# Another order of the weight loads and of the mix stage in a fused attention, soft-MoE and squared-ReLU kernel

## Chip, cores and metric

One Trainium2 chip, one of its cores. The metric is the device time of one launch in microseconds. A profiled execution also has a span, from the first to the last instruction of the trace. TensorE is called PE here, VectorE DVE, ScalarE ACT, GpSimd POOL, and SyncE, which issues most DMAs, SP.

## The reference

Three layers, each on the output of the one before, all in float32, for 4 x 576 = 2304 tokens of 512 features:

```python
# attention, 8 heads of 64, causal window of 128, ALiBi bias
scores = where(mask, q @ k.T / 8 + bias, -1e9)
x = softmax(scores) @ v                      # -> x [2304, 512]
# soft MoE, 8 experts of 4 slots, F = 1024
logits = x @ phi                             # [2304, 32]
slot_input = softmax(logits, axis=0).T @ x   # [32, 512]
slot_out[e] = relu(slot_input[e] @ w1[e]) @ w2[e]
x = softmax(logits, axis=1) @ slot_out       # [2304, 512]
# feed-forward, F = 2048
return relu(x @ w_in) ** 2 @ w_out
```

## The kernel before

All engines run their own program inside one block, and semaphores tie them together.

**Attention** takes 16 steps (4 batches x 4 pairs of heads). SP's loop (lines 401 to 409) issues in step n the v of step n, the k of step n+3, one half of a weight item, and the q of step n+4, all on one queue. PE works on scores, transposes of the probabilities and outputs (lines 938 to 1002; the q transposes are line 921), and the outputs land transposed in `xT`.

**Expert weights** are 16 items of 2 MB: item 2e is w1 of expert e, item 2e+1 its w2. They live in a ring of 8 slots (`RING`, line 31): six in `ring` (`EARLY`), two in `ring_late` at the top of SBUF. `load_half` (line 382) brings items 0 to 5 in twelve halves during attention steps 0 to 11; the first half of item 8, w1 of expert 4, goes to a tile `spare` after the loop (line 410). When the last attention output is done, `load_item` (line 338) brings items 6 and 7. Then come the four loads of w_in (lines 414 to 416, each after four more of the transposed tiles of x, since `win_sb` lies over `xT`), and then the other items in the order of `LATE_ITEMS` (line 34), each when the expert that used its slot is done (`e1_done`, `e2_done`), and last w_out in four loads (line 421).

**Slot inputs.** After attention PE forms the logits (line 1034), transposes x into rows (line 1045), adds up the slot inputs (line 1075), and turns them (line 1106).

**Expert loop** (lines 1162 to 1170). In round e PE does `expert_in(e)` (line 1127, w1), `expert_turn(e-1)` (line 1135), `expert_out(e-2)` (line 1148, w2), and, for the first five, `comb_turn(e-2)` (line 1158), which transposes the softmaxed mixing weights; DVE takes those into `combT` in `take_combT`. After the last expert DVE copies the slot outputs, PE turns them (line 1174) and DVE writes `soT`.

**Mix stage.** The product of slot outputs and w_in, 32 x 2048, is called mix and takes the place of w_in for all tokens. It is formed in four pieces of 512 columns. `mix_parts(n)` (line 1188) makes four partial products, ACT or DVE copies them (`take_part`), `mix_sum(n)` (line 1194) adds them, ACT rounds the sum into `mix` (line 864) and DVE writes the rest for its lower rows (line 708). `MIX_BANKS` names the two PSUM banks of each piece; before, the sum of one piece uses the bank of another's parts. `win_sb` holds w_in with row 4p+c on partition p, so the turn reads the slot outputs with a stride of four, which the copies of lines 632 and 693 put in order.

**Feed-forward.** Blocks of 256 tokens (`FT`), nine in all; a block has eight units u of 256 hidden features. `hidden` (line 1202) is the product of mix and combT for one unit; ACT does relu (line 876) and the rounded square (line 879), DVE the square (line 720) and its lower part (line 724); `project` (lines 1218 to 1220) is three products with the higher and lower parts of w_out, 12 instructions a unit. PE keeps `AHEAD` = 4 units of hidden ahead of the projections. w_out's parts are made in block 0: ACT rounds a unit of `wout_raw` to `wout_hi` (`split_high`, line 854), DVE subtracts (`split_low`, line 689). The order of these on each engine is written out by hand in `first` and `step`. POOL normalizes probabilities in attention (line 467) and clears `hidT`; after that it has nothing to do.

Of the kernel before, what the change touches and what calls it, by code (L numbers as in the profile page):

```python
# [5 lines left out]
F32 = mybir.dt.float32  # L6
F32R = mybir.dt.float32r
ALU = mybir.AluOpType
# [22 lines left out]
RING, RW = 8, 4096  # L31
EARLY = 6
ITEMS = 2 * E
LATE_ITEMS = (8, 10, 12, 9, 14, 11, 13, 15)
SPLIT_ITEM = 8
# [29 lines left out]
def attention_moe_ffn(nc, q, k, v, phi, w1, w2, w_in, w_out, out):  # L65
# [5 lines left out]
    win_v = w_in.rearrange("(p c) f -> c p f", c=DC)  # L71
# [4 lines left out]
    with ctx:  # L76
# [38 lines left out]
        wout_raw = sb("wout_raw", [P, FC, DM])  # L115
        place["at"] = ring_at
# [4 lines left out]
        assert place["at"] == ring_end  # L121

        spare = sb("spare", [P, RW // 2])

# [3 lines left out]
        xT_end = place["at"]  # L128
        place["at"] = xT_at
# [29 lines left out]
        ring_late = sb("ring_late", [P, RING - EARLY, RW])  # L159
# [7 lines left out]
        assert place["at"] <= late_at  # L167
# [9 lines left out]
        place["at"] = comb_end  # L177
        combT = sb("combT", [P, NTOK], F32R)
        assert place["at"] <= late_at
        place["at"] = late_at  # L180
        mix = sb("mix", [P, F2], F32R)
# [24 lines left out]
        spare_loaded = sem("spare_loaded")  # L206
# [74 lines left out]
        wsplit = sem("wsplit")  # L281
        l1_done = sem("l1_done")
# [52 lines left out]
        def ring_slot(slot):  # L335
            return ring[:, slot, :] if slot < EARLY else ring_late[:, slot - EARLY, :]

        def load_item(eng, i):
            e, slot = i // 2, i % RING
            if i >= RING:  # L340
                was = i - RING
                eng.wait_ge(e2_done if was % 2 else e1_done, was // 2 + 1)
            to = ring_slot(slot)
            if i % 2 == 0:
                cols = slice(RW // 2 if i == SPLIT_ITEM else 0, RW)
                eng.dma_start(to[:, cols], w1_v[e][:, cols]).then_inc(ring_loaded[slot], 16)
# [10 lines left out]
        def _(sp):  # L357
# [62 lines left out]
            for i in range(4):  # L420
# [15 lines left out]
        def _(pool):  # L436
# [43 lines left out]
            nc.gpsimd.memset(hidT[:, :, :, :], 0.0).then_inc(hidT_clear, 1)  # L480


        @block.vector
        def _(dve):
# [195 lines left out]
            for e in range(2, E):  # L680
                take_hidT(e)
                if e - 2 < QT:
                    take_combT(e - 2)

            def split_low(u):
# [7 lines left out]
            nc.vector.tensor_copy(slots_sb[:, :].rearrange("r (c x) -> r c x", c=DC),  # L693
                                  psum[:, BK_E2, :].rearrange("r (x c) -> r c x", c=DC)).then_inc(so_ready, 1)
# [16 lines left out]
            take_part(1)  # L711
            split_low(0)
            take_mix(0)
            take_mix(1)


# [12 lines left out]
            def first():  # L729
                low_part(0, 0)  # L730
                take_part(3)
                take_mix(2)
                low_part(1, 1)
                split_low(1)
                low_part(2, 2)
                take_mix(3)
                split_low(2)
                low_part(3, 3)
                split_low(3)

            def step(n, par):
                for u in range(AHEAD, FU):
                    if isinstance(n, int) and n == 0:
                        split_low(u)
                    low_part(FU * n + u, u)
# [11 lines left out]
        def _(act):  # L757
# [108 lines left out]
            take_part(0)  # L866
            split_high(0)
            take_mix(0)
            split_high(1)
            take_part(2)  # L870
            take_mix(1)

# [10 lines left out]
            def first():  # L883
                high_part(0, 0)
                high_part(1, 1)
                take_mix(2)
                split_high(2)
                high_part(2, 2)
                take_mix(3)
                high_part(3, 3)  # L890
                split_high(3)
                split_high(4)

            def step(n, par):
                for u in range(AHEAD, FU):
                    if isinstance(n, int) and n == 0 and u + 1 < FU:
                        split_high(u + 1)
                    high_part(FU * n + u, u)
# [11 lines left out]
        def _(pe):  # L910
# [204 lines left out]
            def expert_in(e):  # L1115
                i = 2 * e
                wait_item(i)
                if e >= 2:
                    pe.wait_ge(hid_ready, e - 1)
                w = ring_slot(i % RING).rearrange("p (c f) -> p c f", c=DC)  # L1120
                early_w = spare[:, :].rearrange("p (c f) -> p c f", c=DC // 2)
                if i == SPLIT_ITEM:
                    pe.wait_ge(spare_loaded, 16)
                for c in range(DC):
                    for j in range(4):
                        w_c = (early_w if i == SPLIT_ITEM and c < DC // 2 else w)[:, c, 2 * P * j:2 * P * j + 2 * P]
                        last = mm(psum[NS * j:NS * j + NS, BK_E1 + e % 2, 0:2 * P], siT[:, c, :], w_c, start=(c == 0), stop=(c == DC - 1))  # L1127
                last.then_inc(e1_done, 1)
# [32 lines left out]

            for e in range(E + 2):
# [4 lines left out]
                if e >= 2:  # L1167
                    expert_out(e - 2)
                    if e - 2 < QT:
                        comb_turn(e - 2)  # L1170

            pe.wait_ge(so_ready, 1)
            for c in range(DC):
                last = mm(psum[:, 1, NS * c:NS * c + NS],
                          slots_sb[:, P * c:P * c + P], fold[:, 0:NS],
                          start=True, stop=True)
            last.then_inc(soT_done, 1)
            pe.wait_ge(soT_ready, 1)


            for c in range(DC):
                pe.wait_ge(win_loaded[c], 16)

            def mix_parts(n):
                if n == 3:
                    pe.wait_ge(mix_ready, 1)
# [19 lines left out]
            def project(n, m, u, par):  # L1206
                pe.wait_ge(lo_done, m + 1)
                if isinstance(n, int) and n == 0:
                    pe.wait_ge(wsplit, u + 1)
# [13 lines left out]
            def first():  # L1223
# [6 lines left out]
                for u in range(AHEAD):  # L1230
                    if u % 2 == 0:
                        pe.wait_ge(mix_ready, u // 2 + 1)
                    hidden(0, u, u)
                    if u == 1:
                        mix_parts(3)
                        mix_sum(2)
                mix_sum(3)

            def step(n, par):
                for u in range(FU):  # L1240
                    if u < FU - AHEAD:
                        if isinstance(n, int) and n == 0:
                            pe.wait_ge(mix_ready, (u + AHEAD) // 2 + 1)
# [11 lines left out]
MIX_BANKS = ((4, 7), (5, 4), (6, 5), (7, 6))  # L1255
# [21 lines left out]
```

## Time and profile before

| | us |
|---|---|
| median of 3 runs | 442.83 (438.8 to 444.55) |
| profiled execution, its own time | 443.9 |
| its span | 441.9 |
| PE busy | 407.4 (92%) |
| DVE busy | 240.2 (54%) |
| ACT busy | 218.9 (50%) |
| POOL busy | 71.6 (16%) |
| mean granted PE clock | 0.98 |

Times in rows are microseconds from the start of the span. "x16" is a count of instructions merged into a row. PE is TensorE's matmuls, PEld its weight loads, SPq the queue of SP. The number in brackets behind a row is the idle time just before it and what ended it. In a row of windows each engine's busy time is followed by its count, then come the granted clock (1.00 is full), the mean busy share of the 16 DMA engines, and GB/s.

### The profile page before, as it was taken

The page shows a single profiled execution, that of the slowest core. Times are in us where ns is not written, and L with a number is a line of the kernel's source. Part 1 is how long each engine was busy: PE and PEld are TensorE (multiplying, and loading weights), DVE is VectorE, ACT ScalarE, POOL GpSimd, SP SyncE. Part 2 cuts the span into 40 slices and gives each one's busy share as a digit, 9 for nine tenths or more (in the row PEclk, how much of TensorE's full clock was granted, in tenths as well). Part 3 has the DMA queues.
Part 4 walks back from the last instruction along what each step waited for, and adds up shares of the span by engine and source line. Part 5 has one row for each costly group of instructions (what it writes and reads, how often), then busy time and mean ns, then how long its engine had stood idle before and what let it go on. Part 6 is the DMA issues. An engine that isn't in the chain of part 4 may idle for free.

```text
span 441.9 us, 7857 instructions
## 1 busy us (share of the span) xinstructions
PE 407.4 (92%) x2851; PEld 307.0 (69%) x2851; DVE 240.2 (54%) x680; ACT 218.9 (50%) x558; POOL 71.6 (16%) x61
## 2 busy tenths in 40 slices
PE   4799999799898988966999999999999999999996
PEld 3578787577676643421278888888888888888884
DVE  3888888687654544200499645454445445455530
ACT  2989889788753320100596434444434434444420
POOL 2374655554450010000000000000000000000000
PEclk9999999999999999986799999999999999999999
DMA  8799999899445969999400101010010101010101
GB/s 163 202 258 248 247 260 239 202 243 258 99 123 188 403 225 406 398 384 386 181 1 2 47 1 47 1 47 0 2 48 1 47 0 47 0 47 0 49 0 47
DMA packets 73411, 61.35 MB, mean 139 GB/s; under 512 B 58785, under 2 KB 58785, under 8 KB 71329
## 3 DMA queue, kind: packets, MB, share of 16 engines
q1 hardware_dynamic: 71264, 60.37, 44.9%
q10 hardware_dynamic: 2112, 0.52, 0.7%
q8 instruction: 21, 0.34, 0.3%
q14 instruction: 14, 0.11, 0.1%
HBM read 56.16 MB, written 4.72 MB: 138 GB/s over the span
## 4 chain that ended last, share of the span: by engine, by line
PE 74%; DMA 11%; SPq 5%; ACT 4%; DVE 3%; POOL 1%; issue 1%; DVEq 0%; ACTq 0%; POOLq 0%
PE psum L1219 15%; PE psum L1220 15%; PE psum L1218 15%; DMA q_in<-in_q 6%; DMA ring_late<-in_moe_w 4%; PE psum L1202 4%; PE psum L951 3%; PE psum L993 3%; PE psum L975 3%; ACT probs L764 3%; PE psum L1127 3%; PE psum L1045 2%; PE psum L1148 2%; PE psum L921 2%; PE psum L1075 1%; PE psum L1188 1%
## 5 line engine op out<-in xcount | busy, mean ns | idle before, releaser
L1220 PE MATMUL psum<-wout_hi,act_lo 128*128 128x512 f32 x288 | 113.3, 394 | 0.0
L1219 PE MATMUL psum<-wout_lo,act_hi 128*128 128x512 f32 x288 | 113.2, 393 | 0.0
L1218 PE MATMUL psum<-wout_hi,act_hi 128*128 128x512 f32 x288 | 112.4, 390 | 0.0
L720 DVE TENSOR_TENSOR sq_h<-relu_h 128x512 f32<-128x512 f32 x72 | 49.7, 691 | 81.5 <-ACT relu_h L876 81.3
L876 ACT ACTIVATE relu_h<-psum 128x512 f32<-128x512 f32 x72 | 43.1, 599 | 91.8 <-PE psum L1202 89.1
L467 POOL TENSOR_TENSOR probs<-probs,row_inv 128x1024 f32<-128x1024 f32 x31 | 59.2, 1929 | 56.2 <-DVE row_inv L558 56.2
L764 ACT ACTIVATE probs<-probs,row_min 128x256 f32<-128x256 f32 (+1 forms) x128 | 60.1, 471 | 13.8 <-DVE row_min L508 13.8
L1220 PEld LDWEIGHTS psum<-wout_hi,act_lo 128*128 128x128 f32 x288 | 54.0, 188 | 11.8
L1219 PEld LDWEIGHTS psum<-wout_lo,act_hi 128*128 128x128 f32 x288 | 54.0, 188 | 10.0
L1218 PEld LDWEIGHTS psum<-wout_hi,act_hi 128*128 128x128 f32 x288 | 54.1, 188 | 9.8
L724 DVE TENSOR_TENSOR act_lo<-sq_h,act_hi 128x512 fp32r<-128x512 f32 x72 | 49.9, 693 | 5.0
L879 ACT ACTIVATE act_hi<-relu_h 128x512 fp32r<-128x512 f32 x72 | 45.6, 633 | 4.3
L508 DVE CUSTOM_DVE_ANT_0 probs<-psum,rel 128x256 f32<-128x256 f32 (+1 forms) x128 | 42.1, 385 | 3.4 <-PE psum L951 3.4
L975 PE MATMUL psum<-ident,probs 128*128 128x128 f32 x224 | 30.3, 274 | 2.5 <-ACT probsT L778 1.4
L1202 PEld LDWEIGHTS psum<-combT,mix 128*128 128x128 f32 x144 | 26.8, 188 | 6.6 <-issue 0.7
L951 PE MATMUL psum<-kT,qT 64*128 64x256 f32 (+1 forms) x256 | 29.8, 373 | 0.0
L1202 PE MATMUL psum<-combT,mix 128*128 128x256 f32 (+1 forms) x144 | 29.2, 286 | 0.0
L550 DVE COPY probsT<-psum 128x512 f32<-128x512 f32 x32 | 22.1, 691 | 11.6 <-PE psum L979 11.2
L993 PE MATMUL psum<-probsT,v_in 128*64 128x256 f32 (+1 forms) x256 | 27.8, 359 | 0.6 <-ACT probsT L778 0.6
L975 PEld LDWEIGHTS psum<-ident,probs 128*128 128x128 f32 x224 | 25.1, 141 | 3.8 <-issue 2.0
L993 PEld LDWEIGHTS psum<-probsT,v_in 128*64 128x64 f32 x256 | 17.3, 136 | 12.3 <-issue 5.6
L951 PEld LDWEIGHTS psum<-kT,qT 64*128 64x128 f32 x256 | 21.5, 194 | 4.7 <-issue 2.5
(131 smaller groups left out, 411.7 us busy)
## 6 DMA issues: line engine op xcount, KB each, us to landing
ring<-in_moe_w SPq DMA_DIRECT2D x13, 1024.0 KB, 6.3
ring<-in_moe_w SPq DMA_DIRECT2D x5, 2048.0 KB, 15.7
ring_late<-in_moe_w SPq DMA_DIRECT2D x3, 2048.0 KB, 14.2
out_x<-out_sb SPq DMA_DIRECT2D x9, 512.0 KB, 2.8
q_in<-in_q SPq DMA_DIRECT2D x32, 128.0 KB, 5.7
v_in<-in_v SPq DMA_DIRECT2D x32, 128.0 KB, 4.3
win_sb<-in_moe_w_in SPq DMA_DIRECT2D x4, 1024.0 KB, 9.7
wout_raw<-in_moe_w_out SPq DMA_DIRECT2D x4, 1024.0 KB, 15.4
```

Source lines behind the costliest of these rows:

```text
L467: nc.gpsimd.tensor_tensor(probs[:, par, h, 0:4, :], probs[:, par, h, 0:4, :], row_inv[:, par, 4 * h:4 * h + 4].unsqueeze(2).to_broadcast([ ...
L720: nc.vector.tensor_tensor(sq_h[:, u % 2, :], relu_h[:, u % 2, :], relu_h[:, u % 2, :], ALU.mult).then_inc(sq_done, 1)
L724: nc.vector.tensor_tensor(act_lo[:, 2 * u:2 * u + 2, :], sq_h[:, u % 2, :].rearrange("p (c t) -> p c t", c=2), act_hi[:, 2 * u:2 * u + 2, ...
L764: nc.scalar.activation(t, t, ACT.Exp, bias=row_min[:, par, one:one + 1], scale=-1.0, accum_out=row_sum[:, par, one:one + 1]).then_inc(exp_ ...
L879: nc.scalar.activation(act_hi[:, 2 * u:2 * u + 2, :], relu_h[:, u % 2, :].rearrange("p (c t) -> p c t", c=2), ACT.Square).then_inc(hi_done, 1)
L951: last = mm(psum[:, score_bank(g, r, h), off + c0:off + 2 * P], qT[rows, two, P * i:P * i + P], kT[rows, two, P * (i - 1) + c0:P * (i + 1) ...
L975: last = nc.tensor.transpose(psum[:, BK_PT + half, at:at + P], probs[:, par, h, i, c:c + P], ident[:, :])
L993: mm(psum[D * h:D * h + D, BK_O, P * j:P * j + w], v_in[:, two, h, j, :], probsT[:, 2 * a[0] + h, a[1]:a[1] + w], start=(j == 0), stop=(j ...
L1202: last = mm(psum[:, u % 4, FT * x:FT * x + FT], mix[:, P * (2 * u + x):P * (2 * u + x) + P], cols, start=True, stop=True)
L1218: mm(to, hi, wout_hi[:, c, :], start=first_of, stop=False)
L1219: mm(to, hi, wout_lo[:, c, :], start=False, stop=False)
L1220: last = mm(to, lo, wout_hi[:, c, :], start=False, stop=last_of)
```

## The change

- The ring has eleven slots (`RING`): seven in `ring` (`EARLY`), slots 7 and 8 in `ring_late` (`LATE`; slot 7 is its upper half), slots 9 and 10 over `xT` (`IN_X`). `spare` is gone.
- SP issues a half in each of attention steps 1 to 14 (items 0 to 6). After attention it loads item 7; items 9 and 10 after eight and sixteen transposed tiles of x; item 8 after the slot inputs, since `e_tok` now reaches into its slot; then items 11 to 15 in order.
- w_in comes behind all expert weights, when expert 4 is done (e2_done 5) and expert 5's first product (e1_done 6), in four loads of 512 columns, of which each piece of the mix waits for its own; the layout is row 128c+p on partition p. w_out's four loads follow at once; `wout_raw` moves to the late slots. `mix` and `combT` move into the seventh ring slot.
- comb is turned from round 4 of the expert loop on (`COMB_FROM`) instead of round 2.
- Five and three transposes of the identity (`keep_warm`) are added before and after the turn of the slot outputs.
- The four pieces of the mix use four bank pairs, 6 and 7, 0 and 4, 2 and 3, and again 6 and 7, and all part products are issued before the second hidden unit.
- Three hidden units, not four, are issued before the first projection; block 0 has an order of its own on PE.
- In block 0 the subtraction of w_out's lower part for units 3, 5 and 7 goes from DVE to POOL. ACT's and DVE's splits in block 0 are interleaved one to a unit.

```diff
+COMB_FROM = 4
+RING, RW = 11, 4096
+EARLY = 7
+LATE, IN_X = (7, 8), (9, 10)
-    win_v = w_in.rearrange("(p c) f -> c p f", c=DC)
+    win_v = w_in.rearrange("(c p) f -> p c f", c=DC)
...
-                if n < 2 * EARLY:
-                    load_half(n // 2, n % 2)
+                if 1 <= n <= 2 * EARLY:
+                    load_half((n - 1) // 2, (n - 1) % 2)
...
-            sp.dma_start(spare[:, :], w1_v[SPLIT_ITEM // 2][:, 0:RW // 2]).then_inc(spare_loaded, 16)
             sp.wait_ge(pv_done, NP)
-            for i in range(EARLY, RING):
-                load_item(sp, i)
-            for c in range(DC):
-                sp.wait_ge(xt_done, B * (c + 1))
-                sp.dma_start(win_sb[:, c, :], win_v[c]).then_inc(win_loaded[c], 16)
-            for i in LATE_ITEMS:
-                load_item(sp, i)
-            sp.wait_ge(e2_done, 5)
+            load_item(sp, LATE[0])
+            for x, slot in enumerate(IN_X):
+                sp.wait_ge(xt_done, 2 * B * (x + 1))
+                load_item(sp, slot)
+            sp.wait_ge(x_used, QT)
+            load_item(sp, LATE[1])
+            for i in range(RING, ITEMS):
+                load_item(sp, i)
...
+            sp.wait_ge(e1_done, IN_X[1] // 2 + 1)
+            sp.wait_ge(e2_done, IN_X[0] // 2 + 1)
+            for i in range(4):
+                load_win(i)
+            for i in range(4):
+                load_wout(i)
...
+            for u in LOWS_OF_POOL:
+                w = slice(2 * u, 2 * u + 2)
+                pool.wait_ge(whigh, u + 1)
+                nc.gpsimd.tensor_tensor(wout_lo[:, w, :], wout_raw[:, w, :], wout_hi[:, w, :].bitcast(F32),
+                                        ALU.subtract).then_inc(wsplit_pool, 1)
...
-                    if e - 2 < QT:
-                        comb_turn(e - 2)
+                    if 0 <= e - COMB_FROM < QT:
+                        comb_turn(e - COMB_FROM)
+            keep_warm(5)
             pe.wait_ge(so_ready, 1)
...
+            keep_warm(3)
             pe.wait_ge(soT_ready, 1)
...
+                mix_parts(3)
+                pe.wait_ge(mix_ready, 1)
+                hidden(0, 0, 0)
+                mix_sum(2)
+                hidden(0, 1, 1)
                 mix_sum(3)
+                pe.wait_ge(mix_ready, 2)
+                hidden(0, 2, 2)
+
+            def first_step():
+                project(0, 0, 0, 0)
+                pe.wait_ge(mix_ready, 3)
+                hidden(0, 3, 3)
+                hidden(0, 4, 4)
+                project(0, 1, 1, 0)
+                hidden(0, 5, 5)
+                project(0, 2, 2, 0)
+                pe.wait_ge(mix_ready, 4)
+                hidden(0, 6, 6)
+                project(0, 3, 3, 0)
+                hidden(0, 7, 7)
+                hidden(1, 8, 0)
+                project(0, 4, 4, 0)
...
+                project(0, 7, 7, 0)
...
-MIX_BANKS = ((4, 7), (5, 4), (6, 5), (7, 6))
+MIX_BANKS = ((6, 7), (0, 4), (2, 3), (6, 7))
+LOWS_OF_POOL = (3, 5, 7)
```

On ACT, and then on DVE, the order around the mix becomes (the loops over u from 2 are in step(0)):

```diff
+            def first():
+                take_part(0)
+                take_mix(0)
+                take_part(2)
+                take_mix(1)
                 high_part(0, 0)
+                split_high(0)
+                take_mix(2)
                 high_part(1, 1)
+                split_high(1)
                 take_mix(3)
...
+                    for u in range(2, FU):
+                        high_part(u, u)
+                        split_high(u)
...
             def first():
+                take_part(1)
+                take_mix(0)
+                take_mix(1)
+                take_part(3)
                 low_part(0, 0)
+                split_low(0)
                 take_mix(2)
                 low_part(1, 1)
                 split_low(1)
                 take_mix(3)
...
+                    for u in range(2, FU):
+                        low_part(u, u)
+                        if u not in LOWS_OF_POOL:
+                            split_low(u)
```

## Rows read from the trace of the kernel before

**Rows 1.** Chain of waits, 170 to 218 us: start, duration, engine and line.
```profile
170.50 1.86 PE psum L1127 x32
172.36 0.37 PE psum L1135 x2
172.73 1.85 PE psum L1148 x16
174.58 0.59 PE psum L1158 x4
...
191.06 15.91 DMA ring_late<-in_moe_w
207.02 1.11 PE psum L1148 x8
...
214.23 2.00 PE psum L1194 x2
216.23 1.09 PE psum L1188 x8
217.32 1.07 PE psum L1194 x2
```

**Rows 2.** PE's timeline, 157 to 224 us: start, duration, instruction, idle before.
```profile
157.22 1.06 PE L1075 MATMUL psum<-x_tok,e_tok 64*32 64x512 f32 x8 [0.81 <-ACT x_tok L822]
...
160.60 3.66 PE L1127 MATMUL psum<-ring,siT 128*32 128x256 f32 x64 [0.38 <-DVE siT L636]
...
169.84 0.66 PE L1158 MATMUL psum<-ident,comb 128*128 128x128 f32 x4 [1.12 <-DVE comb L669]
...
189.52 1.93 PE L1127 MATMUL psum<-ring_late,siT 128*32 128x256 f32 x32 [0.33 <-DMA ring_late<-in_moe_w]
...
194.93 2.71 PE L1148 MATMUL psum<-ring,hidT 128*32 128x512 f32 x16 [3.11 <-DMA ring<-in_moe_w]
...
200.37 3.64 PE L1148 MATMUL psum<-ring,hidT 128*32 128x512 f32 x16 [2.10 <-DMA ring<-in_moe_w]
...
210.59 3.64 PE L1188 MATMUL psum<-win_sb,soT 128*32 128x512 f32 x16 [0.38 <-DVE soT L696]
...
223.16 0.40 PE L1218 MATMUL psum<-wout_hi,act_hi 128*128 128x512 f32 x1
```

**Rows 3.** SP's issues, and the landing of the issue at 162.6.
```profile
141.15 12.70 SPq L416 DMA_DIRECT2D win_sb<-in_moe_w_in  x4
162.60 4.29 SPq L346 DMA_DIRECT2D ring<-in_moe_w  x3
...
ring<-in_moe_w SPq DMA_DIRECT2D x1, 1024.0 KB, 5.0
```

**Rows 4.** Windows: engines' busy time and counts, clock, DMA share, GB/s.
```profile
10.00:17.20 7.20, 5.70 (x43) 4.14 (x41) 5.25 (x30) 5.34 (x22) 1.23 (x1) 1.00 0.65 142
112.00:120.00 8.00, 7.45 (x70) 6.08 (x71) 5.73 (x27) 6.05 (x23) 3.70 (x3) 1.00 0.48 108
196.00:202.00 6.00, 3.90 (x18) 0.69 (x14) 0.19 (x1) 0.00 (x0) 0.00 (x0) 0.50 1.05 387
271.00:295.00 24.00, 24.00 (x114) 19.89 (x113) 11.77 (x17) 10.35 (x17) 0.00 (x0) 1.00 0.06 23
```

**Rows 5.** Waits of PE on q in attention: total, times, longest.
```profile
PE psum L921 <- DMA q_in<-in_q: 11.0, 6, 4.8
```

**Rows 6.** Lines of w_out's split, POOL's and DVE's large products: ns min/median/max.
```profile
L854 ACT CAST wout_hi<-wout_raw x8: 1039/1047/1049, 213.1 to 231.5; 128x1024 fp32r<-128x1024 f32 x8
L689 DVE TENSOR_TENSOR wout_lo<-wout_raw,wout_hi x8: 1215/1218/1224, 214.9 to 238.3; 128x1024 fp32r<-128x1024 f32 x8
...
L467 POOL TENSOR_TENSOR probs<-probs,row_inv x31: 1893/1896/2933, 16.0 to 127.0; 128x1024 f32<-128x1024 f32 x31
...
L561 DVE TENSOR_TENSOR probs<-probs,row_inv x1: 1224/1224/1224, 126.9 to 126.9; 128x1024 f32<-128x1024 f32 x1
```

More of the change, by code:

```diff
@@ L120, in attention_moe_ffn @@
         act_lo = sb("act_lo", [P, FC, FT], F32R)
-        assert place["at"] == ring_end
-        spare = sb("spare", [P, RW // 2])
+        mix = sb("mix", [P, F2], F32R)
+        combT = sb("combT", [P, NTOK], F32R)
+        assert place["at"] >= ring_end
         xT_at = place["at"]
@@ L128, in attention_moe_ffn @@
         xT_end = place["at"]
+        place["at"] = xT_at
+        ring_x = sb("ring_x", [P, len(IN_X), RW])
         place["at"] = xT_at
@@ L158, in attention_moe_ffn @@
         place["at"] = late_at = (att_end - 4 * 2 * RW) // 32 * 32
-        ring_late = sb("ring_late", [P, RING - EARLY, RW])
+        ring_late = sb("ring_late", [P, len(LATE), RW])
+        place["at"] = late_at
+        wout_raw = sb("wout_raw", [P, FC, DM])
         place["at"] = att_at
@@ L166, in attention_moe_ffn @@
         e_tok = sb("e_tok", [P, QT, P])
-        assert place["at"] <= late_at
+        assert place["at"] <= late_at + 4 * RW
         place["at"] = att_at
@@ L335, in ring_slot @@
         def ring_slot(slot):
-            return ring[:, slot, :] if slot < EARLY else ring_late[:, slot - EARLY, :]
+            if slot < EARLY:
+                return ring[:, slot, :]
+            if slot in LATE:
+                return ring_late[:, LATE[1] - slot, :]
+            return ring_x[:, slot - IN_X[0], :]
         def load_item(eng, i):
@@ L678, in take_combT @@
                     ).then_inc(combT_ready, 1)
-            for e in range(2, E):
-                take_hidT(e)
-                if e - 2 < QT:
-                    take_combT(e - 2)
+            for e in range(2, E + 2):
+                if e < E:
+                    take_hidT(e)
+                if 0 <= e - COMB_FROM < QT:
+                    take_combT(e - COMB_FROM)
             def split_low(u):
@@ L734, in first @@
                 split_low(1)
-                low_part(2, 2)
                 take_mix(3)
-                split_low(2)
-                low_part(3, 3)
-                split_low(3)
             def step(n, par):
[L742 to L745, printed above, removed]
+                if isinstance(n, int) and n == 0:
+                    for u in range(2, FU):
+                        low_part(u, u)
+                        if u not in LOWS_OF_POOL:
+                            split_low(u)
+                else:
+                    for u in range(AHEAD, FU):
+                        low_part(FU * n + u, u)
                 if not isinstance(n, int) or n < NFT - 1:
@@ L883, in first @@
             def first():
+                take_part(0)
+                take_mix(0)
+                take_part(2)
+                take_mix(1)
                 high_part(0, 0)
+                split_high(0)
+                take_mix(2)
                 high_part(1, 1)
[L886 to L888 removed]
+                split_high(1)
                 take_mix(3)
[L890 to L892 removed]
             def step(n, par):
[L895 to L898, printed above, removed]
+                if isinstance(n, int) and n == 0:
+                    for u in range(2, FU):
+                        high_part(u, u)
+                        split_high(u)
+                else:
+                    for u in range(AHEAD, FU):
+                        high_part(FU * n + u, u)
                 if not isinstance(n, int) or n < NFT - 1:
@@ L1160, in comb_turn, with keep_warm @@
                 last.then_inc(ct_done, 1)
+            def keep_warm(n):
+                for _ in range(n):
+                    nc.tensor.transpose(psum[:, 0, 0:P], ident[:, :], ident[:, :])
             for e in range(E + 2):
@@ L1208, in project @@
                 if isinstance(n, int) and n == 0:
-                    pe.wait_ge(wsplit, u + 1)
+                    if u in LOWS_OF_POOL:
+                        pe.wait_ge(wsplit_pool, LOWS_OF_POOL.index(u) + 1)
+                    else:
+                        pe.wait_ge(wsplit, u + 1 - sum(x < u for x in LOWS_OF_POOL))
                 if u == 0:
@@ L1229, in first @@
                 mix_sum(1)
[L1230 to L1236, printed above, removed]
-                mix_sum(3)
+                mix_parts(3)
[3 more added lines that the diff above has]
+                hidden(0, 1, 1)
+                mix_sum(3)
+                pe.wait_ge(mix_ready, 2)
[14 more added lines that the diff above has]
+                project(0, 4, 4, 0)
+                hidden(1, 9, 1)
+                project(0, 5, 5, 0)
+                hidden(1, 10, 2)
+                project(0, 6, 6, 0)
+                hidden(1, 11, 3)
+                project(0, 7, 7, 0)
             def step(n, par):
+                if isinstance(n, int) and n == 0:
+                    first_step()
+                    return
                 for u in range(FU):
                     if u < FU - AHEAD:
-                        if isinstance(n, int) and n == 0:
-                            pe.wait_ge(mix_ready, (u + AHEAD) // 2 + 1)
                         hidden(n, FU * n + u + AHEAD, u + AHEAD)
```

49 lines of the change are left out of this document (11 added, 38 removed).

## The prediction

> **What bounds the kernel now.** I read the chain of waits first, then TensorE's (PE's) timeline from 157 us on, then the SP queue with its landings, then windows of clock and DMA share, then the page's groups for the vector work. The chain shows steady expert work in pieces of 1.86 (expert in), 0.37 (turn), 1.85 (expert out) and 0.59 us (mixing weights' turn), and then 15.91 us of one DMA, the last expert weights [rows 1]. The PE timeline shows what that means [rows 2]: the expert loop starts at 160.60, runs without a gap but for 1.12 us before L1158, and then idles 0.33, 3.11 and 2.10 us before L1127 and L1148, each time ended by a DMA. Its second half is bound by loads. In the window from 196 to 202 us the DMA engines are full (share 1.05, 387 GB/s) and the granted clock is 0.50, the 1.2 GHz level, after PE had idled for those 3.11 us [rows 4]. The mix stage starts at 210.59 and the first projection at 223.16 [rows 2]. From there PE works back to back to the end: a block of 256 tokens is eight units and an output copy on each vector engine, and a window of 24 us in the middle has PE busy throughout and just those 17 instructions on ACT and on DVE [rows 4], so 3.0 us to a unit. Nothing of the change touches blocks 1 to 8. So the change has to be read in three places: attention's loads, the expert loads with their order, and the 12.57 us between 210.59 and 223.16 with block 0 behind them.
>
> **Attention.** The waits view charges 11.0 us of PE idle to q_in in 6 waits [rows 5]; the longest, 4.8, is the start of the kernel, so 6.2 us lie in the later steps, where the weight halves (1 MB each) share the SP queue with q, k and v. The change issues no half in step 0 and gives one to each of steps 1 to 14, so up to step 11, where the last q load is issued, there are 11 instead of 12. One half costs 2.7 us of DMA (half of the 5.4 per 2 MB found below). The three halves of steps 12 to 14 fall where the DMA share is 0.48 [rows 4], and each v load has two steps before it is read: nothing. The dropped half stood right behind a stretch at share 0.65 [rows 4], so part of its time may have been free. Gain between 0 and 2.7 us; I take 2.2, because waits that all lie late in the phase are the sign of a queue that falls behind from the start. The spare load's removal frees nothing, since nobody waits behind it. SP itself loses no time: its three new issues lie between waits.
>
> **Expert loads.** First the rate. Three loads of w1 follow each other from 162.60; the first, of 1 MB, lands 5.0 us after its issue, at 167.6 [rows 3]. Items 10, 12, 9 and 14 (8 MB) then land until 189.52, when PE gets w1 of expert 7, item 11 at 194.93 and item 13 at 200.37 [rows 2]. That is (189.5 - 167.6)/4 = 5.5, then 5.4 and 5.4 us for each 2 MB: a full queue, 5.4 us each. Now the new order. Item 7 goes at 136.8, item 9 with the eighth transposed tile. Item 10 goes with the sixteenth, which is when the last of the four w_in loads is issued today, 153.5 [rows 3], and lands alone at 153.5 + 5.0 + 2.7 = 161.2. Item 8 goes when the slot inputs end at 158.3 [rows 2] and lands at 166.6, and from there, with e1_done and e2_done of the first experts met in time, 11, 12, 13, 14 and 15 land at 172.0, 177.4, 182.8, 188.2 and 193.6. Some 4 MB of w_in and 1 MB net of weights no longer stand ahead of them: 13 us of queue.
> What PE would do alone: 8 x (1.86 + 0.37 + 1.85) + 5 x 0.59 = 35.6 us from 160.60, ending at 196.2; the 1.12 us before L1158 goes, as the turns of comb begin two experts later and comb is ready by then. Against the landings: item 8 is wanted at 172.8, item 12 at 182.1, item 13 at 191.9, all early enough; item 14 (expert 7's w1) is wanted at 186.8 and lands at 188.2: a stall of 1.4 us. Item 15 is wanted at 195.7 and has landed. The loop ends at 197.5 instead of 208.13 (L1148's end in the chain [rows 1]): 10.6 us. If DMA is 1 us later than this, so is all that follows, as it is nearly as tight as PE.
>
> **soT and keep-warm.** Today 2.46 us lie between the loop's end and 210.59 at the half clock; at full clock the eight small products take some 0.2 less. The five and three added transposes (about 0.12 us each) lie in PE's idle time while VectorE (DVE) copies. 0.2 us gained, and bounds of 0.5 either way. The mix starts at 197.5 + 2.3 = 199.8.
>
> **w_in and w_out.** They are issued at the end of expert 4's output, about 187.6, with items 14 and 15 still in flight, so the queue stays full: quarters of w_in (2.7 us each) land at 196.3, 199.0, 201.7 and 204.4, w_out's first at 207.1. Wanted are 199.8, 200.9, 203.0 and 205.1, and w_out at 207.8: all just in time. The new w_in rows of 2 KB are of w_out's and w2's kind, which run at 387 GB/s [rows 4]; no row shows them for w_in, and from the slowest window (142 GB/s [rows 4]) to full rate they cost 0 to 18 us; I take 0, by the nearest rows.
>
> **Mix stage.** One part product takes 1.09 and one sum 1.07 us at full clock [rows 1]. From 199.8, called t: parts 0 and 1, sum 0, part 2, sum 1 and part 3 fill PE until t+6.4, then the first hidden pair (0.3). No product waits for a bank now, since the pairs are distinct. ScalarE (ACT) takes 10.35/17 = 0.61 us an instruction there and DVE 11.77/17 = 0.69 [rows 4], so 1.22 for relu and square, until t+8.0; ACT's w_out split of 1047 ns ends at t+9.1 and DVE's half of 1218 ns at t+10.3 [rows 6]. First projection: t+10.4 instead of t+12.57. But only three units are ahead instead of four, and the splits of units 1 to 7 lie in block 0. ACT: 1.22 + 1.05 = 2.3 us a unit against PE's 3.0, enough. DVE from t+10.3 to the last low part it owes: seven of 2 x 0.69, four splits, two mix subtractions of about 0.7, some 16 us, in 21. POOL's three subtractions have no row; the nearest is L467, as large, 1896 ns, which took 2933 ns once, at 127.0, when DVE ran L561, also with two SBUF operands, from 126.9 for 1224 ns [rows 6]. The 1.04 us more are what was left of L561: the two take turns. DVE in block 0 is nearly all such instructions (L689, L720, L724). So the three moved splits save DVE 3 x 1.22 and hold it 3 x 1.9. Walking the units with POOL taking its turn at once, projection 3 starts 0.3 and projection 6 another 1.1 us later than the order allows, and the last projection of the block starts at t+33.6; today it is 12.57 + 21.0 = t+33.6. Without any conflict it is t+32.3; with POOL put off until DVE idles, t+37.9. I take 0, with -1.3 and +4.3 as bounds.
> The Trainium skill (SBUF — State Buffer, on its two separate sides) says that DVE instructions with two SBUF inputs and GpSimd instructions take a shared port pair as "an exclusive lock", whoever starts first holding it for the whole instruction. Our one overlap agrees. By it the +0 case holds if POOL gets in; if the rule were wrong the gain would be 1.3 us larger.
>
> **Sum.** 443.9 - 2.2 - 10.6 - 0.2 - 0.0 = 430.9 for the profiled execution (span 441.9 and 2.0 around it). That execution lies 1.1 above the median of 442.83 (runs of 438.8 to 444.55), so I give 430.5.
>
> **Rivals.** (a) POOL starved: DVE's queue in block 0 never pauses, so POOL gets the port only when DVE runs dry, and projections 3, 5 and 7 wait. For it: DVE's density there; against: attention, where POOL works beside DVE at its plain 1896 ns. 430.5 + 4.3 = 435. (b) Clock: the wait for item 14, or the small products around soT, let the clock fall to 1.2 GHz, as after 194.9 today [rows 2, 4]. Today's mix start at that level took 3.64 us for two parts [rows 2] and 2.00 for a sum, against 2.2 and 1.07 [rows 1]: 2.4 us, and with the expert pieces before it up to 5: 433 to 436. Against it: the gaps are 1.4, 0.8 and 0.4 us; after such gaps at 157 to 160, and after the 1.12 us before L1158, the pieces that followed still took 1.83 to 1.86 us [rows 1, 2], the full clock. (c) Attention gives nothing and the expert queue starts 1 us later: 433.7. (d) Slower than before: quarters of w_in with strided 2 KB rows run like attention's start and not like w2. PE then waits for the fourth quarter at 193.6 + 4.19 MB/rate and at the low clock; the gain of 13.4 is gone once w_in takes 22.5 us in place of 10.8 (13.4 less the clock's 2.4, and 0.7 of slack), 186 GB/s, and at the 142 GB/s of 10 to 17 us [rows 4] the kernel takes 430.5 + 18 + 2.4 - 0.7 = 450. Nothing but the missing row speaks for it. (e) The change doesn't do what it says: e2_done 5 comes after the queue has run dry, so w_in lands 2 us later: 432.5, within the forecast's range.
>
> **Chances.** Forecast (427 to 433.5) 0.61, (a) 0.14, (b) 0.13, (c) 0.10, (d) 0.02. The range 426 to 437 leaves out (d) and the far ends of the others. Two per cent, about what a measurement of this kernel tells from no change, is 434: below it lie nearly all of the forecast (0.59), 0.05 of (a), 0.06 of (b), 0.09 of (c), together 0.79. Slower by over 2% needs (d) at its worst: 0.01 to 0.02.
>
> **What would show it.** Right: PE's expert loop ends at 195 to 198 (less what attention gained), the only DMA idle in it is 1 to 2 us before L1127 of expert 7; clock 1.00 from there to the end; first projection 10 to 11 us after the first mix part; POOL's subtractions take 1.9 to 3.1 us and some DVE instructions near them grow. Wrong: idle before w_in's products by DMA, a clock of 0.50 in the mix, a PE gap of over 3 us in block 0, attention ending no sooner than 136.8.

## The result, and the profile after

The changed kernel takes 429.01 us (median of 4 runs, 426.93 to 433.41) against 442.6 (438.8 to 444.55): ratio 0.968, 95% interval 0.9635 to 0.9728. The longest of the four counts as a slow execution and is not in the ratio. Forecast were 430.5 and a range of 426 to 437. The profiled execution took 426.93 us, with a span of 425.1 against 441.9.

Five marks in PE's timeline cut both spans: the first product of the expert loop, its end, the first product with w_in, the hidden product with which PE enters the step of block 1 (0.23 us before that block's first projection; called the block's start below), and the end.

| stretch, us | before | after | change | forecast |
|---|---|---|---|---|
| start to expert loop | 160.60 | 154.99 | -5.6 | -2.2 |
| expert loop | 47.49 | 38.60 | -8.9 | -10.6 |
| turn of the slot outputs | 2.50 | 2.28 | -0.2 | -0.2 |
| mix stage and block 0 | 36.30 | 35.37 | -0.9 | 0.0 |
| blocks 1 to 8 | 195.04 | 193.87 | -1.2 | 0.0 |

PE's timeline after, which answers to [rows 2] (start, duration, instruction, idle before):

```profile
154.99 5.31 PE L1135 MATMUL psum<-ring,siT 128*32 128x256 f32 x64 [0.38 <-DVE siT L652]
...
184.34 1.93 PE L1135 MATMUL psum<-ring,siT 128*32 128x256 f32 x32 [1.75 <-DMA ring<-in_moe_w]
...
195.87 1.92 PE L1198 MATMUL psum<-win_sb,soT 128*32 128x512 f32 x16
...
206.14 0.47 PE L1231 MATMUL psum<-wout_hi,act_hi 128*128 128x512 f32 x1 [1.47 <-DVE wout_lo L706]
...
231.24 0.40 PE L1212 MATMUL psum<-combT,mix 128*128 128x256 f32 x2
```

One wait for a weight is left in the expert loop, the one before expert 7's w1. But the first 64 products take 5.31 us where they took 3.66. The windows, which answer to [rows 4], say why:

```profile
155.00:160.00 5.00, 5.00 (x64) 2.40 (x64) 1.71 (x4) 1.01 (x2) 0.00 (x0) 0.66 0.94 369
...
196.00:202.00 6.00, 5.91 (x37) 1.21 (x33) 1.83 (x3) 2.34 (x4) 0.00 (x0) 1.00 1.05 387
```

The clock's mean is 0.66 in the first (part of it at 1.2 GHz), and 1.00 where the mix starts; w_in and w_out arrive at 387 GB/s as the other weights do.

PE's waits on q, as [rows 5]; the longest is again the start of the kernel, so 1.1 us are left of 6.2:

```profile
PE psum L932 <- DMA q_in<-in_q: 6.0, 2, 4.9
```

And POOL beside DVE in block 0, from their two timelines (columns as in PE's):

```profile
212.08 2.80 POOL L495 TENSOR_TENSOR wout_lo<-wout_raw,wout_hi 128x1024 fp32r<-128x1024 f32 x1 [57.53 <-ACT wout_hi L868]
```
```profile
211.40 1.22 DVE L706 TENSOR_TENSOR wout_lo<-wout_raw,wout_hi 128x1024 fp32r<-128x1024 f32 x1
212.53 2.89 DVE L730 TENSOR_TENSOR sq_h<-relu_h 128x512 f32<-128x512 f32 x1
```

DVE's L706 ends at 212.62, POOL's product 2.26 us later at 214.88, and DVE's square 0.54 us behind that, at 215.42. Plain, the two take 1.90 us (L467 in [rows 6]) and 0.69 us. So they ran nearly one after the other: 2.8 us for both, where 2.6 is their plain sum. The other two pairs are alike: 3.08 us on POOL, 2.90 and 2.89 on DVE.

### The profile page after: what moved, and what is told of

Read it like the earlier page. It is cut to its first block, busy times and chain, and to the rows that moved or that the text cites. A ratio compares the mean times of both kernels' runs of the same rounds, so it can differ in the third digit from the quotient of the medians.

```text
span 425.1 us, 7869 instructions
## 1 busy us (share of the span) xinstructions
PE 401.8 (95%) x2859; PEld 307.5 (72%) x2859; DVE 242.9 (57%) x677; ACT 218.4 (51%) x558; POOL 80.5 (19%) x64
## 4 chain that ended last, share of the span: by engine, by line
PE 81%; DMA 6%; ACT 4%; DVE 3%; SPq 2%; POOL 1%; issue 1%; ACTq 0%; POOLq 0%
PE psum L1231 15%; PE psum L1232 15%; PE psum L1233 15%; PE psum L962 5%; PE psum L1004 5%; PE psum L986 5%; PE psum L1212 4%; DMA win_sb<-in_moe_w_in 4%; PE psum L1135 3%; ACT probs L778 3%; PE psum L1156 2%; PE psum L1056 2%; PE psum L932 2%; DMA q_in<-in_q 1%; PE psum L969 1%; PE psum L946 1%
## 5 line engine op out<-in xcount | busy, mean ns | idle before, releaser
L1233 PE MATMUL psum<-wout_hi,act_lo 128*128 128x512 f32 x288 | 112.1, 389 | 0.0
L730 DVE TENSOR_TENSOR sq_h<-relu_h 128x512 f32<-128x512 f32 x72 | 56.4, 783 | 78.6 <-ACT relu_h L883 78.5
## 6 DMA issues: line engine op xcount, KB each, us to landing
ring<-in_moe_w SPq DMA_DIRECT2D x4, 2048.0 KB, 11.6
```

The costliest lines, as they stand in the source:

```text
L730: nc.vector.tensor_tensor(sq_h[:, u % 2, :], relu_h[:, u % 2, :], relu_h[:, u % 2, :], ALU.mult).then_inc(sq_done, 1)
L1233: last = mm(to, lo, wout_hi[:, c, :], start=False, stop=last_of)
```

## Experiments

Each ran with the kernel before on its chip. The marks are those of the table, from one profiled execution each; medians of kernels on different chips are compared by their ratio to the kernel before.

**1. The halves alone, on the kernel before.**

```diff
-                if n < 2 * EARLY:
-                    load_half(n // 2, n % 2)
+                if 1 <= n <= 2 * EARLY:
+                    load_half((n - 1) // 2, (n - 1) % 2)
```

> The kernel before with one edit: SP issues the twelve weight halves in attention steps 1 to 12 instead of 0 to 11. Theory (the queue of attention is short of DMA time, and a half dropped ahead of the q loads is worth its 2.7 us or more, since it also stands ahead of every later q): attention's last output ends 2.2 to 5.6 us earlier than in the kernel before on the same chip, the whole kernel about as much, 437 to 440. Rival (the 5.6 us of the changed kernel's profile were a lucky execution; attention's stalls scatter): no change clear of noise, 441 to 443.

439.67 us against 442.41, ratio 0.9942 (0.9911 to 0.9973): 2.6 us, from 1.2 to 3.9. The waits view of this run:

```profile
PE psum L921 <- DMA q_in<-in_q: 5.2, 2, 4.9
```

**2. The halves put back to steps 0 to 13 in the changed kernel.** (The same edit, backwards.)

> The changed kernel with one edit undone: halves in attention steps 0 to 13 instead of 1 to 14. Theory: 2.2 to 5.6 us slower than the changed kernel, 431 to 434, all of it in PE's waits on q_in. Rival (scatter): 429 as the changed kernel.

434.03 us, ratio 0.978 (0.9707 to 0.9852) against 0.968 (0.9635 to 0.9728) for the changed kernel: the way the theory says, but the two intervals overlap a little. The waits view:

```profile
PE psum L932 <- DMA q_in<-in_q: 10.1, 6, 5.0
```

Both speak for the theory, and the rival is partly right too. Without the start's 4.8 to 5.0, PE waits for q 6.2, 5.1 and 2.7 us in the three profiles with halves from step 0 (before, 2, 6), on average 4.7, and 0.3 to 5.1, on average 2.1, in the nine with halves from step 1. The ranges overlap. The edit is worth about 2.6 us; the 5.6 of the profile are that and scatter.

**3. No subtraction on POOL.** `LOWS_OF_POOL = ()`.

> The changed kernel with all eight subtractions of w_out's lower part on DVE, none on POOL. Theory (DVE and POOL take turns on what they share: each of the three POOL subtractions holds one square of DVE for 2.2 us more, 6.6 in all, against 3.7 us that DVE saves): no square is longer than 0.7 us, DVE is freer by 2.9 us in block 0, and block 1 begins about 1 us earlier after the first mix product (34.6 us instead of 35.6); 428. Rival (POOL's help is worth what it was made for): block 1 begins later than 35.6 us after the first mix product, by up to 3.7 us, 430 to 433.

428.93 us, ratio 0.9727 (0.9675 to 0.9779), no difference that can be told by the total. In the profile the stretch from the first mix product to block 1 is 34.7 us (197.23 to 231.92) instead of 35.4, and 35.2 to 35.6 in the other profiles with POOL. DVE's squares are all short again:

```profile
216.21 0.68 DVE L730 TENSOR_TENSOR sq_h<-relu_h 128x512 f32<-128x512 f32 x1
```

So the help of POOL costs about 0.7 us (0.5 to 0.9 by the profiles that it is compared with): each subtraction held DVE for 2.2 us to save it 1.22.

**4. No keep-warm.** Both calls of `keep_warm` removed.

> The changed kernel without the eight added transposes around the turn of the slot outputs. Theory (they lie in idle time and cost nothing, and the clock is at full rate there anyway): the same time within 0.5 us, clock 1.00 in the mix stage. Rival (they keep the clock up): the granted clock falls to 0.50 within a few us of the turn, and the mix stage takes up to 2.4 us more, 431 to 432.

431.7 us, ratio 0.9748 (0.9699 to 0.9798). By the total that isn't the theory's "within 0.5 us", though the interval overlaps the changed kernel's. From the end of the loop to the first projection the profile is the same: 2.28 us for the turn, 10.1 to the first projection, at clock 1.00. The longer span (431.7) is made earlier: expert 7's w1 came late, PE idled for 3.96 us, and the clock fell, 0.50 in a window behind it:

```profile
188.28 3.64 PE L1135 MATMUL psum<-ring,siT 128*32 128x256 f32 x32 [3.96 <-DMA ring<-in_moe_w]
```
```profile
190.00:192.00 2.00, 2.00 (x21) 0.73 (x14) 0.00 (x0) 0.02 (x1) 0.00 (x0) 0.50 1.04 387
```

It comes ahead of the removed transposes, so they can't have caused it. In this one profile the theory holds, neither a cost nor a need; whether they ever hold the clock up isn't shown.

**5. The changed kernel again.**

> The changed kernel unchanged, as the yardstick of the runs beside it and to see what of its profile comes back. Theory: 427 to 431; attention ends anywhere from 131 to 135, the clock at the start of the expert loop is at times 0.50, a unit in blocks 1 to 8 takes 2.98 us again and not 3.00, and POOL's subtractions take 2.8 to 3.1 us. Rival (these were accidents of one execution): a unit takes 3.00 us.

430.85 us, ratio 0.9681 (0.9613 to 0.9749). The clock falls at the start of the loop again (the first 64 products take 5.76 us), POOL takes 2.79 to 3.08, and blocks 1 to 8 take 193.87 us.

**6. The kernel before, with idle PE filled.** 

```diff
+                if e in (5, 6):
+                    keep_warm(20 if e == 5 else 14)
                 wait_item(i)
...
+                        keep_warm(12)
                         pe.wait_ge(last_half_loaded, 16)
...
+            keep_warm(5)
             pe.wait_ge(so_ready, 1)
...
             last.then_inc(soT_done, 1)
+            keep_warm(3)
```

> The kernel before with idle PE filled: 20, 14 and 12 transposes ahead of the three late waits for expert weights, and five and three around the turn of the slot outputs. Nothing else is changed. Theory (of the changed kernel's gain some 2.4 us in the mix stage is only the clock, the rest is the queue): the clock stays at 1.00 from 190 to 217, the expert loop ends no sooner, for it waits for DMA, and the mix stage to the first projection takes 10 to 11 us instead of 12.57; 440. Rival (the pieces after the waits are late because of the clock, so more of the expert loop comes back): the loop also ends over 2 us earlier, 436 to 438.

440.87 us against 444.23, ratio 0.9941 (0.9897 to 0.9985). Its windows, at the half clock before, are at 1.00:

```profile
196.00:202.00 6.00, 3.76 (x32) 2.02 (x32) 0.19 (x1) 0.00 (x0) 0.00 (x0) 1.00 1.04 384
208.80:218.60 9.80, 9.19 (x51) 3.52 (x51) 6.54 (x9) 8.19 (x13) 0.00 (x0) 1.00 0.54 200
```

The loop takes 48.3 us, not less: it was bound by DMA. The mix stage takes 9.8 us to the first projection instead of 12.57, and 33.5 with block 0 instead of 36.3. So some 2.8 us of the kernel before were clock, and at full clock its mix stage and block 0 are 1.8 us shorter than the changed kernel's 35.4.

**7. Half of one load left out.** Half of w1 of expert 6 isn't loaded; old data stand in its place.

```diff
-                eng.dma_start(to, w1_v[e]).then_inc(ring_loaded[slot], 16)
+                cols = slice(0, RW // 2 if i == 12 else RW)
+                eng.dma_start(to[:, cols], w1_v[e][:, cols]).then_inc(ring_loaded[slot], 16)
```

> The changed kernel with half of the load of w1 of expert 6 left out (1 MB; the other half of the slot holds old data, so the output is wrong in expert 6). Theory (the expert loop is bound by DMA by its 1.75 us wait before expert 7's w1, PE by itself coming next): that wait goes, and everything behind it, w_in and w_out included, is 1.4 to 1.8 us earlier, 427.5. Rival (w_out or the vector engines bind behind it): the wait goes, the first projection comes no sooner, 429.

427.23 us, ratio 0.9597 (0.9527 to 0.9668). The wait falls to 0.40 us:

```profile
186.96 1.93 PE L1136 MATMUL psum<-ring,siT 128*32 128x256 f32 x32 [0.40 <-DMA ring<-in_moe_w]
```

That isn't the theory's proof. The loop takes 38.5 us, as without the edit: its first 64 products took 6.53 us, 1.2 more than in the profile after, so PE came that much later to item 14, which itself landed 29.2 us after the loop's start, against 29.3 in the profile after and 29.6 in run 5. A megabyte less ahead of it brought it 0.1 to 0.5 us. The total lies 3.6 us below run 5 on the same chip, twice what the theory gives, with intervals that overlap (0.9613 to 0.9749 there). It goes the theory's way, and neither its size nor its cause is settled.

**8. The clock kept up ahead of the expert loop.** Five transposes before the wait for `si_ready`, three behind the turn.

> The changed kernel with five and three more transposes, ahead of the turn of the slot inputs and behind it, before the expert loop, where its profile shows the clock fall to 0.50 for some 3 us. Theory (the gaps before and in that turn let the clock fall, and its first 64 products then take 5.31 us instead of 3.66): the clock is 1.00 there in every look, the loop starts at the same distance from the last slot input, 427 to 428. Rival (the added products delay the turn or do not hold the clock): no gain, or 0.3 us lost.

430.82 us, ratio 0.9694 (0.9642 to 0.9746): nothing gained. PE's timeline shows why:

```profile
160.69 3.66 PE L1142 MATMUL psum<-ring,siT 128*32 128x256 f32 x64
...
189.46 3.48 PE L1142 MATMUL psum<-ring,siT 128*32 128x256 f32 x32 [2.82 <-DMA ring<-in_moe_w]
```

The clock holds at the loop's start and 1.65 us come back. But item 14 lands only 0.6 us sooner after that start, so the wait for it grows from 1.75 to 2.82. And behind this longer wait the clock falls after all, to 0.50 in the window from 189.4 to 192: expert 7's first products take 3.48 us instead of 1.93. That is 1.65 gained, 1.07 and 1.55 lost, and the loop takes 39.6 us instead of 38.6. The landing of item 14 binds it, and a longer wait there costs clock on top.

**9. Halves in steps 2 to 15.**

```diff
-                if 1 <= n <= 2 * EARLY:
-                    load_half((n - 1) // 2, (n - 1) % 2)
+                if 2 <= n <= 2 * EARLY + 1:
+                    load_half((n - 2) // 2, n % 2)
```

> The changed kernel with the fourteen halves in attention steps 2 to 15 instead of 1 to 14. Theory (each half taken from ahead of the q loads gives attention what it costs in DMA, until the queue no longer falls behind): PE's late waits on q_in, 1.1 to 5.1 us in six looks with halves from step 1, fall below 1 us, and the time falls by 1 to 2 us, 427 to 428. Rival (what is left of the scatter is not the halves but the transfers of q, k and v themselves): waits on q_in as before, 429 to 431.

428.51 us, ratio 0.9728 (0.9668 to 0.9788), which is not clear of the changed kernel's; no late wait on q in this profile, 3.6 us of it in run 10 with the same edit. Theory and rival stay open.

**10. All together.**

```diff
             for x, slot in enumerate(IN_X):
-                sp.wait_ge(xt_done, 2 * B * (x + 1))
-                load_item(sp, slot)
+                for half in range(2):
+                    sp.wait_ge(xt_done, B * (2 * x + half + 1))
+                    load_half(slot, half)
```

with the edits of 3, 8 and 9.

> The changed kernel with four edits: halves in steps 2 to 15; items 9 and 10 in halves, each issued as soon as its own quarter of the transposed tiles is done (4, 8, 12, 16) instead of after 8 and 16; eight transposes around the turn of the slot inputs; no subtraction on POOL. Theory (the six loads from item 10 to item 14 are one chain that starts at the issue of item 10, so an earlier start of item 10 brings item 14, and with the clock kept up PE is early enough to take it): item 14's wait falls below 1 us, the expert loop takes 36 to 37 us instead of 38.5, block 1 starts 34.6 us after the first mix product, attention gives 1 us more; 424 to 426. Rival (the chain is held by item 8's issue after the slot inputs, or by item 12's wait for expert 0): the loop still takes 38 us or more, 427.

427.48 us (424.82 to 430.56), ratio 0.9668 (0.9621 to 0.9714): the lowest ratio of the kernels with a right output and more than one execution, not told apart from the changed one's. Block 1 begins 34.7 us after the first mix product, as foreseen. The loop takes 40.6 us: the rival. The wait for item 14 is 3.85 us, and behind it the clock falls as in run 8 and costs 1.6 us. (Three of the six executions ran at a mean clock of 1.00. Two of them took 424.8 and 424.9 us, as the theory has it, and the third 427.7; what they waited for is not on record.) Windows of DMA share:

```profile
152.00:156.00 4.00, 3.02 (x27) 1.21 (x19) 1.11 (x2) 0.58 (x1) 0.92 (x1) 1.00 0.58 225
156.00:160.00 4.00, 3.98 (x63) 2.71 (x67) 2.07 (x5) 0.68 (x2) 0.88 (x1) 1.00 1.01 344
160.00:164.00 4.00, 4.00 (x64) 1.85 (x60) 2.40 (x6) 1.10 (x3) 0.00 (x0) 1.00 0.79 288
```

The earlier halves only leave the DMA engines with less to do at 152 to 156, until item 8 goes at 155.0, and again before item 12 goes at 165.5, when expert 0's output is done. Item 14 came 21.6 us after item 12's issue, against 19.5 in the profile after.

**11. PE's old order and the old bank pairs** in the mix stage and block 0; ACT and DVE in their new order.

> The changed kernel with the bank pairs and PE's order of the mix stage and block 0 as before: part 3 after the second hidden unit, four units ahead of the first projection. ACT and DVE keep the new order. Theory (with the clock up the old order is no slower, as the kernel before with its idle PE filled took 9.8 us to its first projection): block 1 starts 34.5 to 35.5 us after the first mix product, as in the changed kernel (35.4) or sooner. Rival (the four bank pairs are what shortened this stage): 37 us or more.

431.0 us in its one run. Block 1 begins 36.7 us after the first mix product, between the theory and its rival and nearer to the rival. PE idles 2.33 us before the fifth hidden unit:

```profile
209.84 0.80 PE L1214 MATMUL psum<-combT,mix 128*128 128x256 f32 x2 [2.33 <-DVE mix L724]
210.43 0.63 PE L1233 MATMUL psum<-wout_hi,act_hi 128*128 128x512 f32 x1
```

The third mix piece, which it waits for in this order, is taken by DVE behind w_out's first split. The clock falls behind that gap: six products of the projections start 0.43 us apart instead of 0.23, 1.2 us in all. With w_out arriving this late, the new order is the better one by 1.1 to 1.5 us (35.2 to 35.6 in the other profiles), and most of that is the clock. Order and bank pairs were changed together, but no product waited for a bank.

**12. mix and combT exchanged in their slot.**

> The changed kernel with mix and combT in exchanged places inside the seventh ring slot. From block 1 on the changed kernel takes 1.15 us less than the kernel before in every look (193.87 against 195.02), with the same instructions on all engines. Theory (where mix and combT lie in SBUF decides how fast the weights and the moving rows of hidden are read): the stretch changes again, to anything but 193.87 within 0.05. Rival (their place is of no account): 193.87.

426.79 us in its one run; blocks 1 to 8 take 193.85, as in the changed kernel. The rival.

## Why the prediction was right, point by point

**The whole** was right: 429.01 for 430.5. That it came so close is in part luck. The loop gave 1.7 us less than forecast, and the mix stage and blocks 1 to 8, from which nothing was expected, gave 0.9 and 1.2 more. (The sum itself, 430.9 less the 1.1 by which the profiled execution lay above the median, is 429.8; 430.5 was given.)

**Attention**: forecast 2.2, measured 2.6 (1.2 to 3.9) by run 1. The mechanism holds: a half less ahead of the last q load, its cost in DMA given back. The profile's 5.6 were no test of it.

**Expert loads**: the mechanism was right, the size off. The loop's end at 197.5 meant 36.9 us, and 38.6 were measured. (As the sign of being right it named an end at 195 to 198 less what attention gained, here 189.4 to 192.4; the loop ended at 193.6.) Most of the 8.9 us gained can be read from the rows. Before, PE waited four times for a load: 0.33, 3.11 and 2.10 us [rows 2], and once more in the last expert's second product:

```profile
207.02 1.07 PE L1148 MATMUL psum<-ring_late,hidT 128*32 128x512 f32 x8 [1.30 <-DMA ring_late<-in_moe_w]
```

That is 6.84 us against 1.75 after, 5.1 us less. The 1.12 us before L1158 are gone. And the products from 194.93 to 205.7 lost some 3.5 us to the half clock before, against 1.65 at the loop's start after.

The term that was mis-sized is item 14's landing, forecast 27.6 us after the loop's start. It was 29.3 in the profile after, and 28.7 to 31.5 in the others of the changed kernel and its variants that load all of item 12. The sum took the loads to land strictly one behind the other, 5.4 us each, so 27.0 us from item 10 to item 14. It was 28.6, and not for a pause of the DMA engines:

```profile
155.67:184.29 28.62, 26.91 (x324) 11.46 (x316) 7.88 (x19) 3.31 (x8) 0.00 (x0) 0.95 1.00 380
```

They moved 10.9 MB in that time, at 380 GB/s, where the five loads are 10.5 MB. About 0.7 MB of item 15 was in it, ahead of item 14 (below), less 0.3 MB of item 8 that had come before. That is 1.0 us, and the rate, 380 for 387, makes most of the rest. The stall was 1.75 us for the forecast 1.4, and behind it the loop was as computed (9.25 us for 9.3). The stall stayed small only because PE was late too. The prediction argued from one execution that the short gaps ahead of the loop leave the clock at its full level; it fell there in 11 of the 12 profiles without the extra transposes (the profile before was the twelfth): 5.2 to 6.5 us for 3.66. One execution was taken for a rule. Run 8 shows why this second miss cost little: PE's loss lies in front of the wait for item 14.

**Mix stage and block 0**: forecast 10.4 us to the first projection, measured 10.27; forecast 0 for the whole, measured -0.9. POOL and DVE took turns as the walk assumed, and the last projection of block 0 began 32.6 us after the first mix product (228.49) instead of 33.6. Run 3 prices POOL's part as a whole, conflict less the work that it took from DVE, at a loss of 0.7; the conflict by itself, which the prediction put at 1.3, was not measured. From the first projection to the last of block 0 the walk has 23.2 us, and 22.4 were measured; which of its steps was too long was not taken apart. The Trainium skill says of the shared port pair (SBUF — State Buffer, its two separate sides) that it is an exclusive lock, and that whoever comes first keeps it for the whole instruction. These traces agree: in every pair each instruction was delayed by about the rest of the other's, with some 0.2 us on top.

**What each part of the change is worth**: the late w_in and w_out and the deeper ring carry it, by 8.9 us in the loop and by ending PE's long waits, which also saves the mix stage the half clock (2.8 us by run 6). No run takes the two apart. The new mix stage is 1.8 us longer than the old one at full clock; that this is the price of w_out's late arrival is likely, for its first quarter lands 7.8 us after the first mix product and in run 6 it landed 0.7 us before it, but no run shows it. The later halves give 2.6. The eight transposes gave nothing that run 4 shows.

**The rivals**: (a) POOL starved: no; it got in after the DVE instruction then running. (b) The clock: it fell, but ahead of the loop and not in the mix; behind the wait for item 14 it fell in runs 4, 8 and 10, where that wait was 2.8 to 4.0 us, and cost 1.6 to 2.8 us. (c) Attention gave its share, the queue was late by 1.7 us. (e) No: w_in's issue came 27.1 us after the loop's start, as forecast. (d) No: w_in's 2 KB rows came at the full rate, 387 GB/s with w_out's, and PE waited at most 0.33 us for a quarter in any profile (run 9).

**Blocks 1 to 8** were forecast unchanged and took 1.2 us less. This is unexplained (below). With attention's 2.6 in place of 5.6, the terms give 2.6 + 8.9 + 0.2 + 0.9 + 1.2 = 13.8 us, and the medians differ by 13.6.

## What to carry to other kernels

Draw loads and engine as two clocks and ask at each item which is later: where both are within 2 us of each other, as here, a gain on one is eaten by a wait for the other (runs 8 and 10), and more than eaten where the longer wait lets the clock fall behind it. Only moving both counts. A load pushed behind the ones that are waited for is nearly free until its own consumer is near; what it can cost is the work that must then be done on its arrival. Before a gap is said to leave the clock alone, profile more than one execution. And when a wait gets shorter, ask which of its two ends moved (run 7).

## What the runs showed of the hardware that was not expected

- Blocks 1 to 8 take 195.04 to 195.05 us in the profiles of the kernel before and its variants (before, 1, 6) and 193.84 to 193.87 in those of the changed kernel, at clock 1.00 in both. PE's code there is the same. In the same 120 us four more matmuls are issued, 561 and 565; the windows of before and, under it, of after:

```profile
260.00:380.00 120.00, 120.00 (x561) 99.44 (x561) 58.80 (x85) 51.69 (x85) 0.00 (x0) 1.00 0.06 22
```
```profile
260.00:380.00 120.00, 120.00 (x565) 100.22 (x564) 59.39 (x86) 51.77 (x85) 0.00 (x0) 1.00 0.06 22
```

  The traces show where the time lies: from a product of wout_hi and act_lo to the next of wout_hi and act_hi, PE takes 234 ns from start to start (mean from 260 to 400 us) in the three profiles of the one kind and 227 to 228 in all of the other. There are three such steps to a unit, 192 in the 64 units, and so some 1.3 us; the other steps differ by less and nearly cancel. The four tiles that the projections read (wout_hi, wout_lo, act_hi, act_lo) lie at the same places in both kernels; mix and combT do not. The order within mix's and combT's slot (run 12), the bank pairs and block 0's order (run 11) and POOL's part (run 3) are not the cause. The places of the other tiles weren't tried one by one; it stays open.
- Loads on one queue don't land strictly one after the other. In run 10 DMA moved 11.6 MB from item 8's issue to item 14's landing, though items 8 and 11 to 14 are 10.5 MB: about 1.1 MB of item 15 had gone ahead of item 14, and in the profile after about 0.7 MB.
- Short gaps brought the clock down. Ahead of the loop PE idles 0.81, 0.86 and 0.38 us between small products; the clock fell there in 11 of 12 profiles, and in neither of the two with eight transposes in the last two gaps (runs 8 and 10).
